# A three-block attention and mixer kernel: U's product with a pair's tokens in two fp32r steps, heads two half units earlier, steps reordered

## The reference

```
phi(x)  = concat(exp(p - m), exp(-(p - m)))   p = x @ w_phi (64 x 128), m = row maximum of |p|
attention, per batch and head:  kv = phi(k)^T v,  z = sum phi(k)
                                x = (phi(q) kv) / (phi(q) z + 1e-6)
block 1: u = x + (x^T U V)^T  (U 576 x 32, V 32 x 576);   out1 = u + relu(u w_ch1) w_ch2  (512 x 2048 x 512)
block 2: u = x + (relu(x^T w_tok1) w_tok2)^T              out  = u + relu(u w_ch1) w_ch2  (512 x 1536 x 512)
```

## Time and profile before

| | before |
|---|---|
| median of three runs (lowest, highest) | 985.09 us (984.48, 985.19) |
| profiled execution, its own time | 983.8 us |
| its span in the trace | 981.9 us |
| TensorE matmuls, busy | 963.6 us (98%) |
| TensorE weight loads, busy | 843.9 us (86%) |
| VectorE, ScalarE, GpSimd, busy | 534.8, 318.4, 249.3 us |
| granted TensorE clock | 1.0 of full speed |

### The profile page before, as it was taken

One profiled execution on the slowest core, in us unless ns is written; L12 is line 12 of the kernel. 1 busy time (PEld: TensorE's weight loads), 2 busy tenths in 40 slices (PEclk: granted clock), 3 DMA queues, 4 the chain that ended last, 5 costly groups with the idle time before them and its releaser, 6 DMA issues.

```text
span 981.9 us, 13915 instructions
## 1 busy us (share of the span) xinstructions
PE 963.6 (98%) x5448; PEld 843.9 (86%) x5448; DVE 534.8 (54%) x930; ACT 318.4 (32%) x555; POOL 249.3 (25%) x150
## 2 busy tenths in 40 slices
PE   6999999999999999999999999999999999999998
PEld 6997888878888878888888889988888888888898
DVE  4865887856788757788733333253343343333232
ACT  4654555423444513453420211432211111111111
POOL 3555575713354303444211000650000000000000
DMA  8852222121211211122044103542132123000010
GB/s 206 232 200 74 59 54 68 34 64 46 68 51 53 66 44 53 53 63 54 2 143 117 33 1 125 193 123 81 49 111 73 59 74 90 30 32 12 1 43 23
DMA packets 58272, 72.63 MB, mean 74 GB/s; under 512 B 25696, under 2 KB 41312, under 8 KB 57184
## 3 DMA queue, kind: packets, MB, share of 16 engines
q1 hardware_dynamic: 49840, 62.27, 21.6%
q10 hardware_dynamic: 8368, 9.47, 2.9%
HBM read 57.57 MB, written 14.16 MB: 73 GB/s over the span
## 4 chain that ended last, share of the span: by engine, by line
PE 76%; DVE 2%; issue 1%; ACT 1%; DMA 0%; POOL 0%; SPq 0%; ACTq 0%
PE ps_ring L805 61%; PE ps_m L690 4%; PE ps_m L741 1%; PE ps_ring L621 1%; PE ps_t L664 1%; PE ps_ring L622 1%; PE ps_ring L620 1%; PE ps_a L653 1%; PE ps_a L711 1%; PE ps_a L710 1%; PE ps_a L716 1%; PE ps_t L622 1%; PE ps_t L620 1%; PE ps_t L621 1%; PE ps_a L729 1%
## 5 line engine op out<-in xcount | busy, mean ns | idle before, releaser
L805 PE MATMUL ps_ring<-u_hi,w_hi 128*128 128x512 f32 (+1 forms) x560 | 208.9, 373 | 0.1
L805 PE MATMUL ps_ring<-h_hi,w_hi 128*128 128x512 f32 (+1 forms) x560 | 208.1, 372 | 0.0
L805 PE MATMUL ps_ring<-h_lo,w_hi 128*128 128x512 f32 (+1 forms) x560 | 206.7, 369 | 0.0
L805 PE MATMUL ps_ring<-u_hi,w_lo 128*128 128x512 f32 (+1 forms) x560 | 206.5, 369 | 0.0
L805 PE MATMUL ps_ring<-u_lo,w_hi 128*128 128x512 f32 (+1 forms) x560 | 206.5, 369 | 0.0
L805 PE MATMUL ps_ring<-h_hi,w_lo 128*128 128x512 f32 (+1 forms) x560 | 206.5, 369 | 0.0
L924 ACT ACTIVATE h_hi<-ps_ring 128x512 fp32r<-128x512 f32 (+1 forms) x140 | 77.7, 556 | 372.6 <-PE ps_ring L805 371.4
L1138 DVE SCALAR_TENSOR_TENSOR h_lo<-ps_ring,h_hi 128x512 fp32r<-128x512 f32 (+1 forms) x140 | 88.8, 635 | 198.5 <-ACT h_hi L924 198.4
L1069 DVE TENSOR_TENSOR acc<-ps_ring,acc 128x512 f32<-128x512 f32 (+1 forms) x100 | 63.4, 634 | 108.4 <-PE ps_ring L805 108.1
L805 PEld LDWEIGHTS ps_ring<-u_hi,w_lo 128*128 128x128 f32 x560 | 105.6, 189 | 18.2
L805 PEld LDWEIGHTS ps_ring<-h_lo,w_hi 128*128 128x128 f32 x560 | 105.6, 189 | 18.1
(11 more groups left out here) (147 smaller groups left out, 1210.9 us busy)
## 6 DMA issues: line engine op xcount, KB each, us to landing
kq_raw<-in_k_t SPq DMA_DIRECT2D x55, 160.0 KB, 2.9
w_raw<-in_wa SPq DMA_DIRECT2D x16, 512.0 KB, 6.4
kq_raw<-in_q_t SPq DMA_DIRECT2D x48, 160.0 KB, 2.9
w_raw<-in_wb SPq DMA_DIRECT2D x12, 512.0 KB, 4.0
x_features<-x_scratch SPq DMA_DIRECT2D x4, 1152.0 KB, 6.1
x_by_tokens<-x_turned SPq DMA_DIRECT2D x16, 288.0 KB, 5.4
u_full<-x_scratch SPq DMA_DIRECT2D x4, 1152.0 KB, 6.0
ones_v<-in_v_aug SPq DMA_DIRECT2D x28, 160.0 KB, 2.7
```

The lines of the kernel that those rows point to most:

```text
L805: last = pe.matmul(ps, w, x, start=(k, m) == (0, 0), stop=ended)
```

## The change

1. For the 12 pairs of heads 8 to 31 the product with U is made of fp32r halves. U's two halves stand in columns 0 to 31 and 32 to 63 of `U2`, made once by a new step `split_u` (a copy on ScalarE, a subtraction and a memset on VectorE). The pair's tokens are split too: ScalarE's copies out of `ps_a` now round (`XPH`), and VectorE subtracts that from `ps_a` (`XPL`, in the memory of `DIFF`). `pair_u` multiplies by `XPH` and the new `pair_l` by `XPL`, five matmuls of 64 weight and 128 data columns each. ScalarE copies the result twice, VectorE makes the low rows. The rows of V change to match. The first four pairs stay in fp32.
2. Heads begin at half unit 5 and not 7, `out` comes at offset 8 and not 9, `proj_qt` on TensorE at 3 and not 2. Other offsets of ScalarE, VectorE and GpSimd move by one or two; in particular ScalarE's `prep_k` stands with `exp_k` at 2, GpSimd's `prep_k` at 0 and `prep_q` at 3.
3. The last columns are kept per feature tile, at half units 9, 11, 13 and 15.
4. `STEP_ORDER`, `MIX_AT`, and the order in the prologue (`FIRST_STEPS`, `FIRST_TURNS`, left out below) change. U is loaded in two pieces, 32 and 64 columns wide, and columns 32 to 63 are set to zero by GpSimd.

```diff
-HEADS_AT = [[7, 13, 19, 25, 31, 37, 43, 49], [7, 13, 19, 25, 31, 37, 43, 49], [7, 13, 19, 25, 31, 37, 43, 49]]
+HEADS_AT = [[5, 11, 17, 23, 29, 35, 41, 47], [5, 11, 17, 23, 29, 35, 41, 47], [5, 11, 17, 23, 29, 35, 41, 47]]
 HEAD_STEPS = {
-    "pe": {"proj_k": 0, "proj_qt": 2, "turn_r": 4, "kv": 4, "less_max": 6, "out": 9},
-    "act": {"prep_k": 1, "exp_k": 2, "prep_q": 4, "kv": 5, "less_max": 7},
-    "dve": {"proj_k": 0, "proj_qt": 2, "turn_r": 3, "kv": 5, "out": 9},
-    "pool": {"prep_k": 2, "prep_q": 4, "less_max": 6},
+    "pe": {"proj_k": 0, "proj_qt": 3, "turn_r": 4, "kv": 4, "less_max": 6, "out": 8},
+    "act": {"prep_k": 2, "exp_k": 2, "prep_q": 5, "kv": 4, "less_max": 7},
+    "dve": {"proj_k": 0, "proj_qt": 2, "turn_r": 3, "kv": 5, "out": 8},
+    "pool": {"prep_k": 0, "prep_q": 3, "less_max": 6},
 }
 PAIR_STEPS = {
-    "pe": {"pair_t": 11, "pair_u": 12},
-    "act": {"pair_t": 11, "pair_u": 12},
-    "dve": {"pair_u": 12},
+    "pe": {"pair_t": 11, "pair_u": 12, "pair_l": 12},
+    "act": {"pair_t": 11, "pair_u": 13},
+    "dve": {"pair_t": 11, "pair_u": 13},
...
-MIX_AT = [[27, 45, 51, 61], [27, 45, 51, 61], [27, 45, 51, 61]]
+MIX_AT = [[27, 43, 51, 61], [27, 43, 51, 61], [27, 45, 51, 61]]
...
-                put(16, "save", c)
+                for d in range(DT):
+                    put(9 + 2 * d, "save", (c, d))
...
+                put(4, "split_u", None)
...
-        sp.dma_start(U4[:], u4).then_inc(sem["const_in"], 16)
+        for cols in (slice(0, RANK), slice(2 * RANK, P)):
+            sp.dma_start(U4[:, :, cols], u4[:, :, cols]).then_inc(sem["u4_in"], 16)
...
+        def turned_read(pairs):
+            wait(pe, "xt_copied", pairs)
+            wait(pe, "xl_done", pairs - DT)
...
+                    for t in range(ST):
+                        pe.matmul(xu_bank(n)[0:2 * RANK], U2[:, t, 0:2 * RANK], XPH[:, t, :], start=(t == 0), stop=False)
+            elif name == "pair_l":
+                pe.wait_ge(sem["xl_done"], pn - DT + 1)
                 for t in range(ST):
-                    last = pe.matmul(xu_bank(n), U4[:, t, :], XP[:, t, :], start=(t == 0), stop=(t == ST - 1))
+                    last = pe.matmul(xu_bank(n)[0:2 * RANK], U2[:, t, 0:2 * RANK], XPL[:, t, :], start=False, stop=(t == ST - 1))
                 last.then_inc(sem["xu_done"], 1)
...
-                act.copy(XP[:, 0:FULL].rearrange("p t f -> p (t f)"), xt_banks[:, 0:FULL * P])
-                act.copy(XP[0:S_LAST, FULL], xt_banks[0:S_LAST, FULL * P:]).then_inc(sem["xt_copied"], 1)
+                act.copy(XPH[:, 0:FULL].rearrange("p t f -> p (t f)"), xt_banks[:, 0:FULL * P])
+                act.copy(XPH[0:S_LAST, FULL], xt_banks[0:S_LAST, FULL * P:]).then_inc(sem["xt_copied"], 1)
...
+                    act.copy(H1[0:2 * RANK], xu_bank(n)[0:2 * RANK])
+                    act.copy(H1[2 * RANK:3 * RANK], xu_bank(n)[0:RANK]).then_inc(sem["xu_hi"], 1)
...
                 wait(dve, "kp_done", 2 * n)
+                wait(dve, "xu_done", before_on_dve(("pair_t",), (name, n)) + DT - 1)
...
+            elif name == "pair_t" and not first:
+                dve.wait_ge(sem["kp_done"], 2 * before_on_dve(("proj_k",), (name, n)))
+                dve.memset(XPL[S_LAST:P, FULL].bitcast(F32), 0.0)
+                dve.wait_ge(sem["xt_copied"], pn + 1)
+                dve.tensor_tensor(XPL[:, 0:FULL].rearrange("p t f -> p (t f)"), xt_banks[:, 0:FULL * P],
+                                  XPH[:, 0:FULL].rearrange("p t f -> p (t f)").bitcast(F32), ALU.subtract)
+                dve.tensor_tensor(XPL[0:S_LAST, FULL], xt_banks[0:S_LAST, FULL * P:], XPH[0:S_LAST, FULL].bitcast(F32),
+                                  ALU.subtract).then_inc(sem["xl_done"], 1)
```

More of the change, by code:

```diff
@@ L238 @@
 PIECE = count_pieces()
-SAVES = {(block, c): c + 1 + (0 if block == 1 else B) for block in GROUPS for c in range(B)}
+SAVES = {(block, c): DT * (c + 1 + (0 if block == 1 else B)) for block in GROUPS for c in range(B)}
 W_ORDER = [(block, g, layer, half) for block in GROUPS for g in range(GROUPS[block]) for layer in range(2) for half in range(2)]
@@ L255 @@
 FIRST_TURNS = {
-    "pe": [("kv", 0), ("less_max", 0), ("proj_k", 1), ("proj_qt", 1), ("pair_u", -1), ("out", 0), ("pmix", -2), ("pair_t", -1), ("turn_r", 1)],
-    "act": [("prep_q", 2), ("kv", 0), ("less_max", 0), ("pair_u", -1), ("split_w", -1), ("exp_k", 1), ("prep_k", 3), ("pmix_u", -2), ("pair_t", -1)],
-    "dve": [("proj_k", 1), ("proj_qt", 1), ("pmix", -2), ("pair_u", -1), ("turn_r", 1), ("out", 0), ("split_v4", -1), ("pmix_u", -2)],
-    "pool": [("prep_k", 3), ("prep_q", 3), ("split_w", -3)],
+    "pe": [("kv", 0), ("less_max", 0), ("proj_k", 1), ("pair_u", -1), ("proj_qt", 1), ("out", 0), ("pmix", -2), ("turn_r", 1), ("pair_t", -1)],
+    "act": [("kv", 0), ("less_max", 0), ("split_w", -2), ("exp_k", 1), ("prep_q", 2), ("pair_u", -1), ("prep_k", 3), ("pair_t", -1), ("pmix_u", -2)],
+    "dve": [("proj_k", 1), ("proj_qt", 1), ("pair_u", -1), ("pmix", -2), ("turn_r", 1), ("out", 0), ("split_v4", -1), ("pmix_u", -2)],
+    "pool": [("prep_k", 3), ("split_w", -4), ("prep_q", 3)],
 }
@@ L303, with before_on_dve @@
 DVE_ORDER = [step for c in range(B) for p in range(parts(1)) for step in STEPS["dve"][1, c].get(p, ())]
-assert all(DVE_ORDER.index(("save", n // H - 1)) < DVE_ORDER.index(("out", n)) for n in range(H, B * H))
+assert all(DVE_ORDER.index(("save", (n // H - 1, n % H // 2))) < DVE_ORDER.index(("out", n)) for n in range(H, B * H))
+def before_on_dve(kinds, step):
+    order = PROLOGUE["dve"] + DVE_ORDER
+    return sum(name in kinds for name, n in order[:order.index(step)])
 def before(kinds, step):
@@ L640, in step @@
                 if first:
-                    wait(pe, "xt_copied", before(("pair_t",), (name, n)))
+                    turned_read(before(("pair_t",), (name, n)))
                     for t in range(ST):
@@ L735, in step @@
                     if n == 1:
-                        pe.wait_ge(sem["const_in"], loaded(2))
+                        pe.wait_ge(sem["u4_in"], loaded(2))
+                    for t in range(ST):
+                        last = pe.matmul(xu_bank(n), U4[:, t, :], XP[:, t, :], start=(t == 0), stop=(t == ST - 1))
+                    last.then_inc(sem["xu_done"], 1)
                 else:
@@ L933, in _ @@
                             split_w(what)
+                        elif name == "split_u":
+                            act.wait_ge(sem["xu_done"], DT)
+                            act.copy(U2[:, :, 0:RANK], U4[:, :, 2 * RANK:3 * RANK]).then_inc(sem["u_split"], 1)
                         elif name == "split_wt":
```

57 lines of the change are left out of this document (36 added, 21 removed).

## The result

The changed kernel takes **990.7 us** (median of 4 runs, 990.15 to 991.77), the kernel before 984.96 (4 runs): a ratio of 1.0061, 95% interval 1.0048 to 1.0073. It is 0.6% slower. Forecast were 977.8 us and faster; the range ended at 984.0.

What follows compares the result with a forecast made beforehand. Time was taken as TensorE's work plus what becomes late for it: -4.6 - 6.8 + 2.3 + 1.3 + 0.5 = -7.3 from 983.8 gives 976.5, and 1.3 for the median gives 977.8 us; range 972.5 to 984.0.

Steps and rivals of the forecast that it cites:

- Part 1: U's product on TensorE: ten fp32r matmuls at 0.06 us instead of fp32, saving 0.38 per pair, -4.6 us over 12 pairs.
- C: Rival on U's product: halved weights buy nothing, 0.11 us a matmul, 982.4 us; chance 0.12.
- D: Rival on TensorE: a drain at each change between 64 and 128 weight columns, +7.7, 985.5 us, no change; chance 0.06.
- (c): `pair_l` waiting for VectorE's low half: level in nine turns, 0.15 us late at three chunk ends, +0.5 us.
- Part 2: Chunk ends: heads two half units earlier, `out` at 8, removing TensorE's waits before the transpose and `mix`, -6.8 us.
- (b): `out` at the chunk's end: slack of 0.82 us exceeded by 0.43, three times, +1.3 us.
- (a): `out` waiting for GpSimd's low half of the q features: 0.25 us in each of nine pair turns, +2.3 us.
- Edits at nothing: `exp_k`, last columns' copies, `split_u` (perhaps 0.4 us), starting order, U's load and the k/q loads: nothing in the sum.
- F: Rival: VectorE's new subtraction stretched 2.0 us by GpSimd in 12 pairs, +24, 1002 us, slower; chance 0.05.
- B: Rival: the new waits (4.1 us) don't come and weights go at 0.055, 973 us; chance 0.12.
- E: Rival: k and q loads or GpSimd late, `proj_k` or `out` waits, +5.8, 983.6 us, no change; chance 0.10.
- the loads' loop: Loads of k and q through one buffer: 12.2 us at the shortest in a 13.6 us turn, fitting by 1.4.

Runs made afterwards that it cites:

- run 1: The kernel before with only the new product of U in two fp32r steps, `pair_l` right behind `pair_u`, everything else placed as before: 983.6 us.
- run 8: run 1 with the low half's step behind `less_max` of the same half unit: 982.3 us.
- Run 7: The changed kernel with one more wait on VectorE: its subtraction from the k projection starts only after GpSimd's low half of the head before: 997.3 us.
- Run 10: The changed kernel with the exponentials ahead of the copies of U's product in ScalarE's queue: 981.3 us.
- run 13: Run 10 with the last columns' copies on ScalarE, one half unit later and last in it: 979.6 us.
- run 6: run 5 with `split_u` at half unit 16 of the first chunk instead of 4: 980.6 us.
- run 9: run 6 with the old order of steps ahead of the first chunk and of its turned pair before its product with U: 979.4 us.
- run 4: The changed kernel with `out` back at 9 half units instead of 8 on TensorE and VectorE: 984.4 us.
- run 2: The changed kernel's schedule, heads and saved columns, with U's product in fp32 as before: 991.3 us.
- run 12: run 2 with `out` at 9, at 8 for a chunk's last head, and the old order at the start: 982.3 us.
- run 3: The changed kernel with the last columns' four copies a chunk on ScalarE instead of VectorE: 992.8 us.
- run 11: run 9 with the swap of Run 10 and the first chunk's splits of weights at 39, 49, 52 instead of 42, 48, 49: 977.4 us.
- run 15: run 11 with the last columns' copies moved to ScalarE as in run 13: 977.8 us.
- run 5: run 4 with `out` at 8 for a chunk's last head alone: 981.7 us.
- run 14: Run 10 with `proj_qt` ahead of `out` on VectorE: 982.1 us.

## Why the prediction was wrong

**Part 1 was right.** 0.06 us from start to start for 64 weight columns (57 to 65 ns in 90 of 96, 0.11 in the other six), two steps, no drain: -4.4 against -4.6. C and D fall. But what it is worth depends on what stands between the two steps: 0.35 us in the second and third chunk each with nothing between (run 1), 1.0 with `less_max` between (run 8), as (c) had it for those nine turns. Which of the two edits to the matmul gave the 0.06 is open: the rows at 0.11 were of fp32 with 128 weight columns, the new ones are of fp32r with 64, and no run has the one without the other.

**Part 2 was right** to a tenth: -7.1, of which 0.3 is the matmul's own time, which the table counts with it.

**(b) was right**: 0.29 + 0.1 in each of three, forecast 0.43. **(c)** was level in the nine turns as said; at the ends 0.2 to 0.5 instead of 0.15.

**(a) is the step that failed**, in one term: "it is ready at 328.12 + 2.83", and after the change again 2.83 behind GpSimd's start. The rest of (a) held. (Outside (a), the waits put at nothing are the second failure: below.) With T as the transpose's end (323.79 before, 326.613 - 0.23 = 326.38 after, by the same rule):

| us after T | before | forecast | after |
|---|---|---|---|
| ScalarE's exponentials begin | 2.97 | 3.12 | 3.23 |
| GpSimd's first pass begins | 4.33 | 4.48 | 4.59 |
| its second pass begins | 5.72 | - | 5.98 |
| VectorE's subtraction from the k projection begins | 5.84 | - | 5.51 |
| the low half is ready | 7.16 | 7.31 | 7.99 |
| TensorE wants its second part | 9.49 | 7.07 | 7.19 |

Forecast were 0.24 short, found were 0.80. GpSimd's start is 0.11 late, TensorE's own 0.12 cancels that, and 0.57 is the pass that grew. It did so in nine of nine pair turns: the second pass takes 2.0 us in eight, the first 1.9 in the ninth. The third and fourth rows say why, and I had neither in my sum: before, GpSimd came 0.12 us ahead of VectorE; afterwards VectorE, with the shorter product in front of it, came 0.47 ahead of GpSimd. The later of the two is the one that takes long. The trace of the kernel before had it already, on the other engine: VectorE's subtraction (L984), 0.82 us at its shortest, took some 2.0 in most heads, and one pass of GpSimd, at 189 us, took 2.02. My sum used neither.

```profile
329.63 2.00 DVE L984 TENSOR_TENSOR k_proj_less_max<-k_proj_less_max,k_max 128x640 f32<-128x640 f32 x1
...
L984 DVE TENSOR_TENSOR k_proj_less_max<-k_proj_less_max,k_max x24: 824/1986/2056, 89.4 to 470.3; 128x640 f32<-128x640 f32 x24
```

Run 7 shows that cause alone (passes of 1.43, waits of 0.3, the forecast's size). Run 10 shows the other half: the chain was short of room at all because the exponentials stand behind two copies that nobody is in a hurry for. I had priced that place in the queue (0.15, it was 0.26) and taken it as given. With the 0.1 behind each, nine turns cost 8.6 us instead of 2.3.

**Edits at nothing.** The second failure is a term put at nothing: of the last columns' copies on VectorE the prediction says "nobody behind them is waited for". They took up to 2.7 us (ns, min/median/max over the run; below them the product's subtraction). The earlier trace rows had shown an operation with all operands in SBUF that goes from 0.57 to 2.57 us:

```profile
L1189 DVE COPY u_tail<-u_full x32: 195/277/2735, 96.2 to 909.2; 128x64 f32<-128x64 f32 x8, 128x128 f32<-128x128 f32 x8, 128x192 f32<-128x192 f32 x8, 128x256 f32<-128x256 f32 x8
...
L1072 DVE TENSOR_TENSOR x_pair_lo<-ps_a,x_pair_hi x12: 691/692/692, 126.1 to 498.1; 128x512 fp32r<-128x512 f32 x12
```

I had used that row for VectorE's new subtraction alone (rival F), where it doesn't bear: L1072 has an operand in PSUM and takes 0.69 every time. I did not use it on the copies, where it does. And behind them is waited for: the five operations of `out`, then the block maximum. They cost 3.4 us by the chunks and 1.7 by the medians (run 13, in run 10's schedule). `split_u`, put at 0.4, cost 0.9 (run 6); the order at the start 0.3 in the first chunk (run 9).

**The rivals.** None was the case. B, C, D and F are refuted by the rows above. E came nearest: it said that the loop of loads or GpSimd would be late and that `proj_k` or `out` would wait. `proj_k` never waits for a load in the chunks, but `out` does wait for GpSimd, and for 10.5 us and not the 5.8 that E gave it; E named no cause for that and had a chance of 0.10. F had the sign and the culprit pair, GpSimd and VectorE, and the wrong operation.

**The sum again**, with what the runs gave: -4.4 - 7.1 + 1.2 for the ends' products, +1.2 for (b), +8.6 for (a) in nine turns, +3.4 for the copies, and a rest of +3.4: +6.3, and 0.9 ahead of the first chunk. Of the rest 0.9 is `split_u`, 0.3 the order at the start, 0.9 a late `out` at 476 us (gone in run 10), and 1.0 a wait of `turn_r` at 154 us, which goes only with `out` at 9 (run 4); its cause was not isolated.

The slack of the loads' loop was off too, without effect: two rounds of 3.4 + 0.72 + 1.6 are 11.4 us at the shortest, and not 12.2.

## What to carry to other kernels

A duration from a row holds only with its neighbours: before you carry one of GpSimd or VectorE over, work out which of the two starts first after the change. When a step is moved so far forward that its margin is gone, look in each queue of its chain for work ahead of it that nobody is waiting for: one swap on ScalarE gave 9.4 us here, more than the change was forecast to bring. And a gain on the bounding engine is only what its followers can keep: in four schedules the same product was worth -1.3, 0.1, 1.2 and 1.6 us by the chunks of one execution each (runs 2, 1, 9 with 12, and 8), and 0.6, 1.0, 2.9 and 2.6 by the medians, never the 4.6 of TensorE's work alone.

## What the hardware showed that I had not expected

**Who starts first keeps the other out.** GpSimd's pass over 128x576 takes 1.43 us alone and 2.02 behind VectorE's subtraction. That subtraction takes 0.83 alone. It takes 1.2 when it begins 0.5 us before GpSimd's first pass ends and so gets in ahead of the second, and 2.0 when it begins 0.1 us into the second. Both times it ends 0.68 us behind the end of the pass that it met: 333.09 after 332.41 in the changed kernel, 331.63 after 330.95 in the one before. A scalar operation on 64x18 elements (L1059) took 0.17 and up to 2.14: twice it began 0.07 us ahead of a GpSimd operation of over 2 us and kept its 0.17, and each of the eleven times that it began within one it took 0.24 or more. Small copies of four sizes took 0.28 in the median and up to 2.7.

The Trainium skill, SBUF — State Buffer, section SBUF: two separate sides, says that VectorE and GpSimd share one pair of ports as a lock, held for a whole instruction by whichever starts first, and it counts among VectorE's operations those with two SBUF inputs and those in a two-port mode. The traces agree: in each of these cases the one that starts first keeps its time and the other ends late. They can't show the mode of the scalar operation and the copies. They agree on the operand in PSUM too: in the changed kernel L1072 hardly meets GpSimd (0.1 us at most), but in runs 4 and 9 one lies wholly within a GpSimd operation and takes 0.692 like the rest, and `h_lo`'s (L1180, the same form as the earlier trace rows) never takes over 0.693 in 140 times, 34 of them beside GpSimd for more than half of their time.

**Work that is sooner can make others later.** With the shorter product VectorE reached its subtraction 0.33 us sooner after the transpose, and got in ahead of GpSimd. With the old product in the same schedule (run 2) the passes of eight of the nine pair turns took 1.4 us each; the ninth took 2.02, and that is the one wait left there.

**A product of 64 weight columns** with 128 columns of data goes at 57 to 65 ns a matmul (granted clock 1.00 in the chunks). The Trainium skill, TensorE: Matmul & The Clock Gate, section Wait — 56ns, not 53.3ns?, gives 55.6 ns for 128 columns of data at the higher clock; the trace is 1 to 9 ns above that.

**The start varies by itself.** With the same steps there, runs 9 and 12 reach the first chunk at 68.78 and 70.68 us. From 15 to 17 us TensorE starts 19 matmuls in one and 11 in the other, though both rows show a granted clock of 1.00; the short ones follow each other at 0.112 and at 0.213 us (the two windows, of run 9 and of run 12):

```profile
15.00:17.00 2.00, 2.00 (x19) 2.00 (x18) 0.00 (x0) 0.79 (x2) 1.00 (x1) 1.00 1.01 293
```

```profile
15.00:17.00 2.00, 2.00 (x11) 2.00 (x11) 0.00 (x0) 0.00 (x0) 1.12 (x1) 1.00 0.83 260
```

Why is open. It is not all chance, though. Over all the profiles the 61st matmul starts at 18.67 us (run 2) to 20.32 (run 3). Behind it the executions are steadier. From there to the first chunk take 49.90 to 49.93 us the five runs with the new product and the old order of steps (1, 8, 9, 11, 15), 50.36 and 50.37 the kernel before and run 12, and 50.38 to 51.42 the nine with the new order (the changed kernel and runs 3 to 7, 10, 13, 14). The four longest of these nine, 51.00 and up, are those in which TensorE waits 0.4 to 0.8 us for the values' load. So the new order does cost 0.5 to 1.5 us there, as run 9's theory had it, and of the 1.9 us between runs 9 and 12 0.46 is not chance: the kernel before differs from run 1 by as much, so it may be U's load in two pieces, which was not tried alone.
